# Two more tiles of the output stage turned by VectorE's blocks and on-chip transfers instead of TensorE

## The reference

```
attn: q, k, v [8, 8, 576, 64]; k and v are mean-pooled over groups of 8 rows (72 keys);
      softmax(q k^T / 8) v, heads joined to x [4608, 512]
moe:  logits = x phi [4608, 32]; d = softmax over tokens; slot_input = d^T x;
      8 experts: relu(slot_in w1) w2 -> slot_out [32, 512]
      c = softmax of logits over the 32 slots; x = c slot_out
moe2: h = x w_in                       [4608, 1024]
      e = exp(h - max h); solu = h * e / (sum e + 1e-9)
      ln = (solu - mean) / sqrt(var + 1e-6) * g_ln
      out = ln w_out                   [4608, 512]
```

## Time and profile before

| | |
|---|---|
| median of three executions | 476.89 us |
| the profiled execution, its own time | 478.42 us |
| its span | 476.6 us |
| TensorE busy, share of the span | 93% |
| VectorE, ScalarE, GpSimd busy | 67%, 53%, 53% |
| mean granted TensorE clock | 0.98 of full speed |
| output stage (first h matmul to the end) | 245.5 to 476.6 us |

### The profile page before, as it was taken

The page is one execution under the profiler, slowest core; times in us unless marked ns, Lnnn a source line. Parts: engine busy times, 40 slices in busy tenths (PEclk is TensorE's granted clock), DMA queues, the critical chain, the costliest instruction groups (busy, mean ns, idle before and its releaser), DMA issues.

```text
span 476.6 us, 9885 instructions
## 1 busy us (share of the span) xinstructions
PE 442.9 (93%) x3468; PEld 350.6 (74%) x3468; DVE 319.9 (67%) x534; ACT 253.8 (53%) x550; POOL 254.6 (53%) x346
## 2 busy tenths in 40 slices
PE   1897999999999998799859999999999999999996
PEld 0876888888888885344438887878788888888885
DVE  7655777768777774654557997767677777777411
ACT  2356567586766764303427765555556555555310
POOL 0396777888678522012114334656666666666540
PEclk9998899999999999999987999999999999999999
DMA  8969598988979564999900126666666666666652
GB/s 264 300 147 286 200 283 293 315 224 289 264 274 297 188 222 171 376 371 399 387 19 1 44 46 136 133 124 136 125 133 136 133 136 134 134 133 135 134 125 46
DMA packets 125342, 91.70 MB, mean 192 GB/s; under 512 B 104824, under 2 KB 104832, under 8 KB 123264
## 3 DMA queue, kind: packets, MB, share of 16 engines
q1 hardware_dynamic: 125312, 91.32, 69.6%
HBM read 66.13 MB, written 9.44 MB: 159 GB/s over the span
## 4 chain that ended last, share of the span: by engine, by line
PE 72%; SPq 12%; DVE 6%; DMA 3%; ACT 3%; issue 3%; POOL 1%; DVEq 0%
SPq L437 10%; PE banks L1442 9%; PE banks L1443 9%; PE banks L1444 9%; PE banks L1110 8%; PE banks L1162 5%; PE banks L1098 4%; PE banks L1178 3%; PE banks L1326 3%; PE banks L1142 3%; PE banks L1214 3%; PE banks L1346 3%; PE banks L1419 3%; PE banks L1186 2%; PE banks L1118 1%
## 5 line engine op out<-in xcount | busy, mean ns | idle before, releaser
L1442 PE MATMUL banks<-wo_hi,uh 128*128 128x512 f32 x288 | 112.8, 392 | 0.0
L1443 PE MATMUL banks<-wo_lo,uh 128*128 128x512 f32 x288 | 112.4, 390 | 0.0
L1444 PE MATMUL banks<-wo_hi,ul 128*128 128x512 f32 x288 | 112.1, 389 | 0.0
L545 POOL TENSOR_TENSOR ul<-u_col,uh 128x1024 fp32r<-128x1024 f32 x30 | 72.1, 2405 | 33.7 <-ACT uh L574 33.7
L471 POOL TENSOR_TENSOR attn<-attn,srec 128x576 f32<-128x576 f32 (+1 forms) x40 | 45.9, 1147 | 62.4 <-DVE srec L827 62.4
L760 ACT ACTIVATE sq<-u,usum 128x1024 f32<-128x1024 f32 x36 | 41.5, 1152 | 41.7 <-DVE u L1031 41.7
L1444 PEld LDWEIGHTS banks<-wo_hi,ul 128*128 128x128 f32 x288 | 54.2, 188 | 11.3
L1442 PEld LDWEIGHTS banks<-wo_hi,uh 128*128 128x128 f32 x288 | 54.2, 188 | 11.2
L1443 PEld LDWEIGHTS banks<-wo_lo,uh 128*128 128x128 f32 x288 | 54.2, 188 | 11.1
L1021 DVE TENSOR_REDUCE nmax<-banks 128x1 f32<-128x1024 f32 x36 | 43.5, 1219 | 18.5 <-PE banks L1419 18.4
L1110 PE MATMUL banks<-kblk,qT 128*128 128x144 f32 (+1 forms) x320 | 51.7, 309 | 4.5 <-issue 2.4
(11 more groups left out here) (158 smaller groups left out, 731.4 us busy)
## 6 DMA issues: line engine op xcount, KB each, us to landing
wslot<-in_moe_w SPq DMA_DIRECT2D x14, 2048.0 KB, 10.2
u_col<-u_blk SPq DMA_DIRECT2D x240, 64.0 KB, 2.1
qb<-in_q SPq DMA_DIRECT2D x32, 256.0 KB, 6.3
out<-osb SPq DMA_DIRECT2D x32, 256.0 KB, 2.5
kraw<-in_k SPq DMA_DIRECT2D x8, 640.0 KB, 7.9
vraw<-in_v SPq DMA_DIRECT2D x8, 640.0 KB, 5.2
kraw<-in_k SPq DMA_DIRECT2D x8, 512.0 KB, 6.3
vraw<-in_v SPq DMA_DIRECT2D x8, 512.0 KB, 4.0
```

Source lines behind the costliest of these rows:

```text
L545: pool.tensor_tensor(ul[par][:, :, :].rearrange("p c (q t) -> p (c q) t", q=4), v, uh[par][:, :, :].bitcast(F32).rearrange("p c (q t) -> p ...
L1442: pe.matmul(ps[4 + par], uh[par][:, c, :], wo_hi[:, c, :], start=(c == 0), stop=False)
L1443: pe.matmul(ps[4 + par], uh[par][:, c, :], wo_lo[:, c, :], start=False, stop=False)
L1444: last = pe.matmul(ps[4 + par], ul[par][:, c, :], wo_hi[:, c, :], start=False, stop=(c == FC - 1))
```

## The change

`LEAD` goes from 6 to 4: only tiles 0 to 3 are turned by TensorE, tiles 4 and 5 by blocks and transfers. `moved`, the count of landed transfers that `hi_col` and `blocks` wait for, is adapted to a first pair (4, 5) in slot 0, and SyncE's first `shuffle` is issued in step 0 instead of step 2. The loops of TensorE, ScalarE and VectorE now hold steps 4 to 27 and eight steps are written out behind them.

```
-LEAD = 6
+LEAD = 4
...
         def moved(x, k):
-            return (x - k % 4) * 64 - (256 if k % 4 < 2 else 0)
+            return (x - k % 4) * 64
...
             def out_step(i, k, base):
                 if not (isinstance(i, int) and i == 0):
                     store(i - 1, k - 1, base)
-                if k % 2 == 0 and not (isinstance(i, int) and (i < 2 or i + AHEAD >= OUT_TILES)):
+                if k % 2 == 0 and not (isinstance(i, int) and i + AHEAD >= OUT_TILES):
                     shuffle(i + 4, k + 4)
```

## The result

| | before | changed |
|---|---|---|
| median of 12 executions each | 476.24 us | 481.04 us |
| ratio, 95% interval | | 1.0109 [1.0087, 1.0130] |
| span of the profiled execution | 476.6 us | 478.3 us |
| its own time | 478.42 us | 480.14 us |
| mean granted TensorE clock | 0.980 | 0.976 |

The change costs about 1.1%: 4.8 us between the medians, 5.2 by the ratio. The two profiled executions show only 1.7 us of it.

The account below looks back on a forecast made before the run. SyncE's DMA queue, nearly tied with TensorE, was taken to bound the output stage: one more pair (11.63 us), started 7.24 earlier, makes it 4.4 us late. 476.89 + 4.4 = 481.3 us, range 479.0 to 484.2.

Parts of the forecast that it names:

- The start of the new pair and the queue's delay: SyncE's queue: pair (4, 5) starts at 270.91 us; pair (6, 7) and every later pair come 4.4 us late.
- The wait at step 4: TensorE stands still about 5 to 6 us before step 4, whose matmuls can begin at 287.2 to 288.1 us.
- the later u(5): VectorE, step 1: two added block transposes make u(5) 1.2 us later; TensorE loses some 0.5 to 0.9 us there.
- had its cover: Tile 9 ready for pair (8, 9) at 293 us, queue there at about 294 to 295.4; costed at nothing.
- The clock: TensorE behind the step 4 wait: lower clock level loses 1.8 us, fitting into its 2 to 3 us lead; no cost.
- it is again the queue that is waited for: Up to step 14 the queue limits TensorE, which gets 2 to 3 us of small waits between steps 5 and 14.
- rival B: Queue pauses fall elsewhere: 480.3 us with one gone, 478.4 to 479.3 with two, one more adds 5.6; chance 0.28.
- one of the prediction's own signs of being wrong: Step 14 of TensorE released by nothing, which would point to the clock or TensorE instead of the queue.
- rival C: Low clock lasts longest after the step 4 wait, 5.5 us lost; 4.9 to 7.9 us on the sum; chance 0.20.
- Rival A: Turned tiles are in time, no wait at step 4; saved transposes and removed waits give 472.8 us; chance 0.04.
- Behind step 14: Nothing changes behind step 14, so the delay stays 4.4 us on the whole span.

Follow-up runs that it names:

- extra_pair: Kernel before, TensorE's transposes kept, with block transposes and the 16-DMA shuffle of tiles 4 and 5 added to no use; ratio to before 1.0106.
- assist4: Changed kernel with 5 of the first pair's 16 DMAs issued on ScalarE's queue instead of SyncE's; ratio to before 1.0026.
- fill: Changed kernel with 16 unused matmuls on TensorE behind the output of tile 3, where it waits for tile 4; ratio to before 1.0076.
- one_dma: Changed kernel with the first pair (4, 5) moved by one straight DMA instead of 16, its outputs not turned rightly; ratio to before 1.0032.
- lead8: LEAD = 8: first eight tiles turned by TensorE, 16 more transposes than the kernel before; ratio to before 1.0045.

## Why the prediction was right

The forecast was 481.3 us in 479.0 to 484.2; the median is 481.04. Its base has since moved from 476.89 to 476.24, so the difference is 4.8 us, or 5.2 by the ratio, where 4.4 was forecast. The start, the wait and what bounds it were forecast rightly; that the two medians agree within 0.3 us is luck, and so in part is the size, as one of its steps was off.

- **The start of the new pair and the queue's delay.** Forecast 270.91, which is 9.71 us after step 1 of the trace of before; measured 269.21 - 259.50 = 9.71. The pair (6, 7) 4.4 us late; measured 4.47. extra_pair shows that the added pair costs 1.06% even where nothing depends on it, assist4 that the issue time is the cause.
- **The wait at step 4.** Forecast 5 to 6 us and step 4 at 287.2 to 288.1, or 26.0 to 26.9 after step 1; measured 25.63. Idle before step 4 were 4.16 us. From the pair's start to step 4 it took 15.92 us, less than the 16.3 to 17.2 that I had taken from other pairs (no pause, 10.55 us on the queue), and h of tile 7 had already waited 0.67 for the later u(5), as forecast. The pair (8, 9) had its cover: the blocks of tile 9 end at 291.68, and the queue came to it at 293.97.
- **The clock.** It fell to its lower level for a part of step 4, as after the row 34.3 to 37.7 of the earlier trace rows, and cost 7.56 - 5.89 = 1.67 us for the 1.8 forecast. The Trainium skill (TensorE: Matmul & The Clock Gate, section HAM oscillation), by which the clock is low behind long waits for a DMA between bursts of matmuls, agrees with this wait. Behind the small waits of fill and one_dma, 0.6 to 1.1 us, the clock stayed at 1.00, and steps take 6.0 us. The prediction read the section as if it held for such waits too; its example is of long ones.
- **The step that was off: "it is again the queue that is waited for".** I took the clock's loss as hidden under 2 to 3 us of queue waits up to step 14. In the two traces those waits are 0.65 and 0.1 us. TensorE came out of step 4 with the clock's 1.67 us on it, and was then behind the queue for most steps. The queue's limit came down a little too: up to the pair (14, 15) it lost 1.4 and 0.7 us to pauses (291.38, 316.05) where it had lost 1.3 and 1.2, and the pause ahead of the pair (16, 17), with the late landing beside it, was gone, as rival B had it. Step 14 starts 86.9 and 86.3 us after step 1, and nothing holds it there, which was one of the prediction's own signs of being wrong; the forecast's 344.59 + 4.4 is 87.8. So this stretch was set by the clock and by the queue together, at nearly the forecast's size: fill removes the clock's part, and in its trace the queue's waits take its place.
- **A sum that was wrong:** rival C lets TensorE reach step 14 at 349.5 to 350.5. With 5.5 us lost it gets there at 346.1 to 347.0 + 5.5 = 351.6 to 352.5; that 2 to 3 of them are hidden under the queue's delay does not bring it there earlier. C's case is thus 7.0 to 7.9 us, not 4.9 to 7.9. The measured loss of 1.67 us is far from either.
- **Rival A** (the tiles are in time) is excluded: even with the transfers shrunk to one issue step 4 waits 1.1 us.
- **Behind step 14** the prediction saw nothing. Steps are about 5.89 in both kernels up to step 30, but step 34 waits for the queue again and the end is 0.2 and 0.7 us later, a difference the prediction had listed as a sign of being wrong.

What stays open: by the times the loss is 4.8 to 5.2 us; from step 1 to the end the traces of the changed kernel take 218.8 and 218.7 us, those of before 215.4 and 213.8, which is 3.3 to 5.0. Why the pauses of before differ in length between its two traces is not shown, nor whose program the q8 reads fetch.

## What to carry to other kernels

Work taken off the busiest engine pays only if what replaces it is ready in time: count the issues on the queue it goes to, from the moment their input exists, and add what is queued behind them. A queue that is as long as the bound engine's step (11.63 against 11.78 us here) has no room for one more item, and if the engine's last steps are shorter than the others it is waited for again at the end; help is worth most on the first one, where the queue is behind, and a helper's issues are free only where they run beside its own work and wait for nothing.

## What the runs showed of the hardware

- A DMA issue on ScalarE's queue ran beside its activation: two issues of 1.42 us in total and an activation of 1.12 us begin together in assist4.
- SyncE's queue lost 0.6 to 1.9 us at places that go with reads on the instruction queue q8 (0.02 MB each). The first read behind the loop moved with the loop's end (406 to 412 us in lead8, 436 to 446 in the changed kernel). That the read causes the pause is not shown. The third of the pauses of before (337.93) has a read too, and a landing of 3.38 us (337.27) instead of 2.1 lies across it.
- The issue of a 1 MB copy between on-chip tensors holds the queue 0.52 us (one_dma, L436), against 0.65 us for each of the 64 KB blocks: here the hold goes with the count of issues, not with the bytes.
